# Attention output stored features-first: 1/total spread along TensorE's columns instead of turning tiles in a three-stage float32 kernel

## The chip, the cores and the metric

One NeuronCore of a Trainium2 chip runs the whole program. The metric is the device time of one execution in microseconds, as the median over runs; 1,080.85 us before the change.

## The reference, cut to what matters

Three stages follow each other, all in float32:

```python
# attention: batch 4, heads 8, sequence 576, head size 64
scores = q @ k.T / 8 + bias                      # bias from a small network on positions
attn = exp(scores - max); attn /= attn.sum(-1) + 1e-09
x = (attn @ v) as [2304 tokens, 512 features]    # token = batch*576 + s, feature = head*64 + d
# dense layer, 512 -> 2048 -> 512
h = x @ w_in;  g = h - tanh(h);  x2 = g @ w_out
# routing to one of 8 experts, 512 -> 1024 -> 512
out[token] = gate * (relu(x2 @ w1[e]) @ w2[e])
```

## The kernel before, in words

**Attention.** Two heads at a time form a pair; there are 16 pairs (`PAIRS_A`), and pair `g` belongs to batch `g % 4`. The 576 queries of a pair are five tiles (`QT`): four of 128 and one of 64 (`rows`). The loop over `STEPS` runs one step per pair and tile, written by hand and in software-pipelined order on each engine. In one step TensorE does, in this order: the scores of the next tile (L412, 12 matmuls), the transposes of the probabilities into `pt_a` (L420, four), one slot of the product with v for the pair before (L427, two float32 matmuls of 512 columns, one for each head: the first writes partitions 0 to 63 of the output, the second 64 to 127), the transposes into `pt_b` (four), one `turn_out` (L458), and the transpose of the middle tile of probabilities into `misc`. In the last step of a pair (tile 4) `values_rest` stands between `turn_out` and that last transpose: ten float32 matmuls of 64 columns in the same two-head form.

The product with v leaves the output turned: partitions are the 128 features of the two heads, columns are tokens. VectorE copies it to `o_sb` (`copy_main` L672, `copy_rest` L678). `turn_out` then transposes one tile of `o_sb` into a quarter of the bank `misc`, and `scaled` (L664) multiplies it by 1/total, which `inverse` (L650 to L654) has computed as [token, tile, head], and writes `x_sb`. SyncE stores each pair's `x_sb` in `x_dram` [token, feature] with two DMAs (L368, L369). `misc` has one user at a time: `misc_free` makes TensorE wait for ScalarE's copy of the middle tile, for `copy_rest` and for `scaled`.

**The passage to the dense layer.** After the last step TensorE turns the first chunk of x (`turn_first_x`, L929, 12 transposes into the three free score banks), turns tiles 1 to 4 of pair 14, finishes the product with v for pair 15, does `first_up` (the first two up-projections, L985), turns the five tiles of pair 15, and enters the dense loop.

**Dense layer.** Six chunks of 384 tokens (`CHUNKS`, `CN`), 16 slots each (`FT`, one per 128 of the 2048 hidden features), so 96 slots. In a slot `m` TensorE does up-projection `m + 2` (12 matmuls of 384 columns, L985) and down-projection `m` (9 matmuls of 512 columns, L1042). Every operand is split in a high and a low part; `g` goes ScalarE, VectorE, ScalarE, VectorE before the down-projection may start (L1149 to L1256; `low`, L1230, comes last). At slots 0, 3 and 6 of a chunk (`X_PREP`) `turn_x` transposes one 128-token tile of the next chunk of x (four transposes, L1029); ScalarE and VectorE split it into `xt_hi` and `xt_lo` (L1142, L1235). At slots 1, 3, 5, 7 and 9 of chunk 0 both also split 1 MB of weights (L1178, L1180, `split_w`). x is loaded into `x_nat` by three DMAs per chunk (L891).

**Experts.** Gather, two matmul layers, scatter; not touched, save for the name of a semaphore.

## Time and profile before

| | |
|---|---|
| median of 3 runs | 1080.85 us (1079.69 to 1084.35) |
| profiled execution | 1080.45 us, its span 1078.7 us |
| TensorE matmul busy | 1037.8 us (96%) |
| TensorE weight load busy | 819.0 us (76%) |
| VectorE busy | 680.2 us (63%) |
| ScalarE busy | 626.1 us (58%) |
| GpSimd busy | 91.2 us (8%) |
| mean granted TensorE clock | 0.989 of full speed |

A busy share is a mean over stages with different limits, and matmuls are pipelined, so a busy TensorE is not one at its peak; what a change is worth is read from the distance between the starts of instructions in the stage that it touches. One float32 matmul shows as two records in the trace; a float32 transpose, or a matmul of rounded (fp32r) operands, as one.

### The profile page before, as it was taken

The page shows a single profiled execution, that of the slowest core. Times are in us where ns is not written, and L with a number is a line of the kernel's source. Part 1 is how long each engine was busy: PE and PEld are TensorE (multiplying, and loading weights), DVE is VectorE, ACT ScalarE, POOL GpSimd, SP SyncE. Part 2 cuts the span into 40 slices and gives each one's busy share as a digit, 9 for nine tenths or more (in the row PEclk, how much of TensorE's full clock was granted, in tenths as well). Part 3 has the DMA queues.
Part 4 walks back from the last instruction along what each step waited for, and adds up shares of the span by engine and source line. Part 5 has one row for each costly group of instructions (what it writes and reads, how often), then busy time and mean ns, then how long its engine had stood idle before and what let it go on. Part 6 is the DMA issues. An engine that isn't in the chain of part 4 may idle for free. (4 is left out here: it accounts for less than half of the span.)

```text
span 1078.7 us, 19176 instructions
## 1 busy us (share of the span) xinstructions
PE 1037.8 (96%) x6642; PEld 819.0 (76%) x6642; DVE 680.2 (63%) x1544; ACT 626.1 (58%) x1331; POOL 91.2 (8%) x134
## 2 busy tenths in 40 slices
PE   5879999999999999999999999999999999999995
PEld 2246666666665899999999999999987888888884
DVE  7967777777787796656657657668753452631410
ACT  6977777777787676655556556556631442622321
POOL 0000000000000000000100100001021331331311
PEclk9999999999999999999999999999989999999998
DMA  6772252431503430000000100201115351531110
GB/s 215 263 243 57 56 177 68 165 84 51 167 24 103 166 108 30 1 30 30 31 1 30 31 1 30 79 30 47 48 40 191 127 200 39 198 110 40 36 47 25
DMA packets 69043, 92.14 MB, mean 85 GB/s; under 512 B 25035, under 2 KB 36683, under 8 KB 68939
## 3 DMA queue, kind: packets, MB, share of 16 engines
q1 hardware_dynamic: 63706, 79.32, 22.5%
q0 software_dynamic: 4192, 11.07, 3.1%
q8 instruction: 51, 0.84, 0.3%
q10 hardware_dynamic: 1056, 0.61, 0.2%
q14 instruction: 38, 0.30, 0.1%
HBM read 66.19 MB, written 25.73 MB: 85 GB/s over the span
## 5 line engine op out<-in xcount | busy, mean ns | idle before, releaser
L985 PE MATMUL score<-dl_xt,dl_weights 128*128 128x384 f32 x1152 | 220.6, 339 | 0.0
L985 PEld LDWEIGHTS score<-dl_xt,dl_weights 128*128 128x128 f32 x1152 | 201.9, 188 | 5.0
L563 ACT ACTIVATE at_prob<-at_neg,at_negmax 128x576 f32<-128x576 f32 (+1 forms) x160 | 123.8, 774 | 52.7 <-DVE at_negmax L644 43.6
L1149 ACT ACTIVATE dl_val<-score 128x384 f32<-128x384 f32 x96 | 47.1, 491 | 145.6 <-PE score L985 144.9
L1239 DVE SCALAR_TENSOR_TENSOR dl_sq<-dl_sq,dl_val 128x384 f32<-128x384 f32 x96 | 53.5, 557 | 111.6 <-ACT dl_sq L1151 111.5
L644 DVE CUSTOM_DVE_ANT_0 at_neg<-score,at_bias 128x576 f32<-128x576 f32 (+1 forms) x160 | 113.9, 748 | 5.6 <-PE score L412 5.3
L1764 PE MATMUL o_acc<-dl_weights,ex_ht_hi 128*128 128x512 f32 (+1 forms) x336 | 108.9, 405 | 1.9 <-DVE ex_ht_lo L1855 1.9
L1733 PE MATMUL score<-dl_weights,ex_xt_hi 128*128 128x512 f32 x336 | 107.3, 401 | 1.4 <-DVE ex_xt_lo L1855 1.4
L427 PE MATMUL o_acc<-at_prob_t,at_v_nat 128*64 128x512 f32 (+1 forms) x320 | 85.7, 616 | 1.2 <-DVE at_o_sb L672 1.2
L1448 POOL DMA_INDIRECT slot_dram<-slot_rows,slot_i x18 | 18.1, 1006 | 750.4 <-DVE slot_i L1320 746.0
L420 PEld LDWEIGHTS pt_b<-id_sb,at_prob 128*128 128x128 f32 (+1 forms) x320 | 32.4, 141 | 63.2 <-ACT at_prob L563 47.8
L1764 PEld LDWEIGHTS o_acc<-dl_weights,ex_ht_hi 128*128 128x128 f32 x336 | 62.5, 191 | 16.0 <-issue 2.1
L1733 PEld LDWEIGHTS score<-dl_weights,ex_xt_hi 128*128 128x128 f32 x336 | 62.7, 192 | 14.0 <-DVE ex_xt_lo L1855 1.8
L1855 DVE TENSOR_TENSOR ex_ht_lo<-pt_b,ex_ht_hi 128x512 fp32r<-128x512 f32 x21 | 14.5, 691 | 89.8 <-ACT ex_ht_hi L1804 89.8
L1816 ACT ACTIVATE ex_y_sb<-o_acc,dl_tile_rows 128x512 f32<-128x512 f32 x21 | 14.4, 688 | 97.1 <-PE o_acc L1764 97.1
L1764 PE MATMUL o_acc<-dl_weights,ex_ht_lo 128*128 128x512 f32 (+1 forms) x168 | 66.8, 398 | 0.0
L1733 PE MATMUL score<-dl_weights,ex_xt_lo 128*128 128x512 f32 x168 | 66.4, 395 | 0.0
L412 PE MATMUL score<-at_k_hi,at_q_hi 64*128 64x288 f32 x320 | 58.6, 342 | 4.8 <-DVE at_negmax L644 3.2
L1042 PE MATMUL o_acc<-dl_weights,dl_g_hi 128*128 128x512 f32 x192 | 60.3, 395 | 2.5 <-DVE dl_g_lo L1230 2.5
L1151 ACT ACTIVATE dl_sq<-dl_val,minus_b 128x384 f32<-128x384 f32 x96 | 59.3, 618 | 3.1
L1042 PE MATMUL score<-dl_weights,dl_g_hi 128*128 128x512 f32 x192 | 59.8, 392 | 0.0
L1250 DVE COPY_PREDICATED dl_sq<-dl_over,dl_big 128x384 f32<-128x384 uint32 x96 | 57.7, 601 | 3.3
(214 smaller groups left out, 2123.5 us busy)
## 6 DMA issues: line engine op xcount, KB each, us to landing
dl_raw<-in_moe_w SPq DMA_DIRECT2D x12, 1024.0 KB, 7.0
ex_raw_b<-in_moe_w SPq DMA_DIRECT2D x8, 1024.0 KB, 6.3
at_bias<-bias_dram SPq DMA_DIRECT2D x3, 2304.0 KB, 10.1
bias_dram<-at_prob SPq DMA_DIRECT2D x20, 288.0 KB, 2.1
at_k_all<-in_k SPq DMA_DIRECT2D x16, 288.0 KB, 3.5
at_q_all<-in_q SPq DMA_DIRECT2D x16, 288.0 KB, 4.3
at_v_nat<-in_v SPq DMA_DIRECT2D x16, 288.0 KB, 3.1
bias_dram<-at_rows_sb SPq DMA_DIRECT2D x16, 288.0 KB, 3.7
```

Of the source, the lines that this page charges most:

```text
L412: last = nc.tensor.matmul(score[c][:, half, 0:HALF], a[g % 2][part, cols], b[g % 2][part, keys], start=i == 0, stop=i == 2)
L427: last = nc.tensor.matmul(o[c * D:(c + 1) * D, at:at + queries.stop - queries.start], v_nat[g % NV][keys, j, :], prob_t[g % 2][keys, j, qu ...
L563: nc.scalar.activation(prob[n % 2][0:m, c, :], neg[c][n % 2][0:m, :], ACT.Exp, bias=negmax[c][n % 2][0:m, 0:1], scale=-1.0, accum_out=tota ...
L644: nc.vector.tensor_tensor_reduce(out=neg[c][n % 2][0:m, :].rearrange("p (a c) -> p a c", a=2), in0=score[c][0:m, :, 0:HALF], in1=bias[hp % ...
L985: last = nc.tensor.matmul(h_ps[m % NHB][:, 0:CN], w[f // KT][:, k, fc], x[c % 2][:, k, :], start=k == 0 and n == 0, stop=k == KT - 1 and n ...
L1042: last = nc.tensor.matmul(x2_ps[j][:, :], g[m % 2][:, tok], w[f // KT][:, f % KT, :], start=f == 0 and n == 0, stop=f == FT - 1 and n == 2)
L1149: nc.scalar.activation(val[m % 2][:, :], h, ACT.Square).then_inc(act_step, 1)
L1151: nc.scalar.activation(sq[m % 2][:, :], val[m % 2][:, :], ACT.Square, bias=minus_b[:, 0:1], scale=SQ_A).then_inc(sq_done, 1)
L1239: nc.vector.scalar_tensor_tensor(out=sq[m % 2][:, :], in0=sq[m % 2][:, :], scalar=SQ_C, in1=val[m % 2][:, :], op0=ALU.add, op1=ALU.mult).t ...
L1250: nc.vector.copy_predicated(s[:, :], over[m % 2][:, :].bitcast(mybir.dt.uint32), big[m % 2][:, :]).then_inc(dve_step, 1)
L1733: last = nc.tensor.matmul(h_ps[half][:, :], x[:, k, :], w1_of(r, half, w)[:, k, :], start=k == 0 and n == 0, stop=k == KT - 1 and n == 2)
L1764: last = nc.tensor.matmul(y_ps[:, :], x[:, half * KT + k, :], w2_of(half, w, k), start=half == 0 and k == 0 and n == 0, stop=half == 1 and ...
```

## The change

x is kept with features on rows all the way. `turn_out` becomes `turn_inverse`: in the same place of TensorE's order, two float32 matmuls per tile instead of one transpose. The stationary operand is one column of 1/total read 64 times (step 0), the moving one the identity, so each lays 1/total of one head along the columns of 64 partitions. `scaled` multiplies `o_sb` by it. `x_dram` becomes [feature, token]; the store is one DMA per pair, the load one DMA per chunk, straight into the form the up-projection wants. `turn_first_x` and `turn_x` are gone; ScalarE and VectorE split x from SBUF (`split_x_high`, `split_x_low`). `load_x` of a later chunk waits for `xt_ready` where it waited for `turned`.

```diff
-        x_sb = [buf(f"x_sb{i}", [P, QT, 2 * D]) for i in range(2)]
+        x_sb = [buf(f"x_sb{i}", [P, QT * 2 * D])[:, 0:S] for i in range(2)]
...
-        x4 = x_dram[0:TOK, :].rearrange("(b s) (c e) -> b c s e", b=NB, e=2 * D)
+        x4 = x_dram.rearrange("(c e) (b s) -> b c e s", b=NB, e=2 * D)
...
-                    dst = x4[p % NB, p // NB]
-                    sp.dma_start(dst[0:MAIN, :].rearrange("(t p) d -> p t d", p=P), x_sb[p % 2][:, 0:QT - 1, :]).then_inc(x_out[p % 2], 16)
-                    sp.dma_start(dst[MAIN:S, :], x_sb[p % 2][0:LAST, QT - 1, :]).then_inc(x_out[p % 2], 16)
+                    sp.dma_start(x4[p % NB, p // NB], x_sb[p % 2]).then_inc(x_out[p % 2], 16)
...
-            def turn_out(p, tile, bank, at):
+            def turn_inverse(p, tile, bank, at):
+
                 if tile == 0:
-                    pe.wait_ge(o_read, p + 1)
-                if tile == QT - 1:
-                    pe.wait_ge(rem_read, p + 1)
+                    pe.wait_ge(norm_step, 2 * p + 2)
                 m = rows(tile)
-                nc.tensor.transpose(bank[0:m, at:at + P], o_sb[:, tile * P:tile * P + m], id_sb[:, :]).then_inc(turn_done, 1)
+                for c in range(2):
+                    one = inv[p % 2][0:m, tile, c:c + 1]
+                    many = bass.AP(one.tensor, one.offset, [one.ap[0], [0, D]])
+                    last = nc.tensor.matmul(bank[c * D:(c + 1) * D, at:at + m], many, id_sb[0:m, 0:m], start=True, stop=True)
+                last.then_inc(turn_done, 1)
...
-            dense.turn_first_x(pe)
             misc_free(PAIRS_A, 0)
             for tile in range(1, QT - 1):
-                turn_out(LASTP - 1, tile, misc, tile * P)
+                turn_inverse(LASTP - 1, tile, misc, tile * P)
...
             def scaled(p, tile, tiles, bank, at):
...
-                dve.wait_ge(norm_step, 2 * p + 2)
                 dve.wait_ge(turn_done, QT * p + tile + tiles)
...
+                dve.wait_ge(o_read, p + 1)
+                if tile + tiles == QT:
+                    dve.wait_ge(rem_read, p + 1)
+                nc.vector.tensor_tensor(x_sb[p % 2][:, cols], o_sb[:, cols], bank[:, at:at + m], ALU.mult).then_inc(x_done, tiles)
...
         def load_x(sp, c):
-            for j in range(CH):
-                sp.dma_start(x_nat[:, j, :], x_tiles[c, :, j, :]).then_inc(x_in[j], 16)
+            sp.dma_start(x_t, x_dram[:, c * CN:(c + 1) * CN].rearrange("(k p) t -> p k t", p=P)).then_inc(x_in, 16)
...
         def load_second_x(sp):
-            sp.wait_ge(turned, CH)
+            sp.wait_ge(xt_ready, CH)
             load_x(sp, 1)
...
+        def split_x_high(act, c, j):
             cols = slice(j * P, (j + 1) * P)
+            act.wait_ge(x_in, 16 * (c + 1))
+            if c >= 2:
+                act.wait_ge(h_done, FT * (c - 1))
+            nc.scalar.activation(xt_hi[c % 2][:, :, cols], x_t[:, :, cols], ACT.Copy).then_inc(xt_high, 1)
+
+        def split_x_low(dve, c, j):
+            cols = slice(j * P, (j + 1) * P)
+            dve.wait_ge(xt_high, c * CH + j + 1)
+            nc.vector.tensor_tensor(xt_lo[c % 2][:, :, cols], x_t[:, :, cols], xt_hi[c % 2][:, :, cols].bitcast(F32),
                                     ALU.subtract).then_inc(xt_ready, 1)
...
                 down(m)
-                j = x_prep(m)
-                if j is not None:
-                    if m == 0:
-                        attention.turned(pe)
-                    turn_x(m // FT + 1, j)
                 j = x2_turn(m)
...
-    x_dram = scratch("x_dram", (TOK, DM))
+    x_dram = scratch("x_dram", (DM, TOK))
```

In the order of the built programs, TensorE, one step of the attention loop from the `pt_a` transposes on (output<-operands, size, how many in a row; `at_inv` is 1/total). Before:

```order
L420 MATMUL pt_a<-id_sb,at_prob 128x128 x4
L427 MATMUL o_acc<-at_prob_t,at_v_nat 64x512 x2
L420 MATMUL pt_b<-id_sb,at_prob 128x128 x4
L458 MATMUL misc<-id_sb,at_o_sb 128x128
L420 MATMUL misc<-id_sb,at_prob 128x128
```

and now:

```order
L416 MATMUL pt_a<-id_sb,at_prob 128x128 x4
L423 MATMUL o_acc<-at_prob_t,at_v_nat 64x512 x2
L416 MATMUL pt_b<-id_sb,at_prob 128x128 x4
L456 MATMUL misc<-id_sb,at_inv 64x128 x2
L416 MATMUL misc<-id_sb,at_prob 128x128
```

One transpose among transposes has become two matmuls of 64 partitions, in the same place. TensorE again, from the last step of attention into the dense loop. Before:

```order
L458 MATMUL misc<-id_sb,at_o_sb 128x128
L427 MATMUL misc<-at_prob_t,at_v_nat 64x64 x10
L420 MATMUL misc<-id_sb,at_prob 128x64
L929 MATMUL score<-id_sb,dl_x_nat 128x128 x12
L458 MATMUL misc<-id_sb,at_o_sb 128x128 x3
L458 MATMUL pt_a<-id_sb,at_o_sb 64x128
L427 MATMUL o_acc<-at_prob_t,at_v_nat 64x512 x8
L427 MATMUL pt_b<-at_prob_t,at_v_nat 64x64 x10
L985 MATMUL score<-dl_xt,dl_weights 128x384 x24
L458 MATMUL misc<-id_sb,at_o_sb 128x128 x4
L458 MATMUL pt_a<-id_sb,at_o_sb 64x128
L985 MATMUL score<-dl_xt,dl_weights 128x384 x12
```

and now:

```order
L456 MATMUL misc<-id_sb,at_inv 64x128 x2
L423 MATMUL misc<-at_prob_t,at_v_nat 64x64 x10
L416 MATMUL misc<-id_sb,at_prob 128x64
L456 MATMUL misc<-id_sb,at_inv 64x128 x6
L456 MATMUL pt_a<-id_sb,at_inv 64x64 x2
L423 MATMUL o_acc<-at_prob_t,at_v_nat 64x512 x8
L423 MATMUL pt_b<-at_prob_t,at_v_nat 64x64 x10
L974 MATMUL score<-dl_xt,dl_weights 128x384 x24
L456 MATMUL misc<-id_sb,at_inv 64x128 x8
L456 MATMUL pt_a<-id_sb,at_inv 64x64 x2
L974 MATMUL score<-dl_xt,dl_weights 128x384 x12
```

The 12 transposes of the first chunk, which stood ahead of the first reuse of `misc`, are gone, and the turns of pairs 14 and 15 are twice as many instructions. TensorE, end of slot 0 of the dense loop. Before:

```order
L1042 MATMUL pt_b<-dl_weights,dl_g_hi 128x512 x2
L1042 MATMUL pt_b<-dl_weights,dl_g_lo 128x512
L1042 MATMUL score<-dl_weights,dl_g_hi 128x512 x2
L1042 MATMUL score<-dl_weights,dl_g_lo 128x512
L1029 MATMUL misc<-id_sb,dl_x_nat 128x128 x4
L985 MATMUL score<-dl_xt,dl_weights 128x384 x12
```

and now:

```order
L1020 MATMUL pt_b<-dl_weights,dl_g_hi 128x512 x2
L1020 MATMUL pt_b<-dl_weights,dl_g_lo 128x512
L1020 MATMUL score<-dl_weights,dl_g_hi 128x512 x2
L1020 MATMUL score<-dl_weights,dl_g_lo 128x512
L974 MATMUL score<-dl_xt,dl_weights 128x384 x12
```

The four transposes are gone here and in 14 more slots; nothing stands in their place.

## Rows read from the trace of the kernel before

**Rows 1.** Stretches: engine busy us (instructions), granted clock, DMA share, GB/s

```profile
98.00:344.00 246.00, 244.25 (x2106) 153.19 (x2106) 193.12 (x573) 185.07 (x521) 0.00 (x0) 1.00 0.34 100
360.00:762.00 402.00, 401.50 (x2137) 365.24 (x2138) 275.26 (x553) 249.45 (x497) 14.25 (x15) 1.00 0.12 41
```

**Rows 2.** Timeline, TensorE matmuls, attention: start us, us, engine, line, count

```profile
301.65 0.40 PE L412 MATMUL score<-at_k_hi,at_q_hi 64*128 64x288 f32 x2
...
305.15 0.40 PE L412 MATMUL score<-at_k_hi,at_q_hi 64*128 64x288 f32 x2
...
312.34 0.40 PE L412 MATMUL score<-at_k_hi,at_q_hi 64*128 64x288 f32 x2
...
315.73 0.40 PE L412 MATMUL score<-at_k_hi,at_q_hi 64*128 64x288 f32 x2
...
319.16 0.40 PE L412 MATMUL score<-at_k_hi,at_q_hi 64*128 64x288 f32 x2
```

**Rows 3.** The same timeline, one step from its `pt_a` transposes on

```profile
309.94 0.65 PE L420 MATMUL pt_a<-id_sb,at_prob 128*128 128x128 f32 x4
310.53 1.08 PE L427 MATMUL o_acc<-at_prob_t,at_v_nat 128*64 128x512 f32 x4
311.54 0.66 PE L420 MATMUL pt_b<-id_sb,at_prob 128*128 128x128 f32 x4
312.03 0.27 PE L458 MATMUL misc<-id_sb,at_o_sb 128*128 128x128 f32 x1
312.14 0.27 PE L420 MATMUL misc<-id_sb,at_prob 128*128 128x128 f32 x1
```

**Rows 4.** The same, a narrow window at 310.5 us: the first two of those four L427

```profile
310.53 0.65 PE L427 MATMUL o_acc<-at_prob_t,at_v_nat 128*64 128x512 f32 x2
```

**Rows 5.** The same timeline, last step of a pair

```profile
307.75 0.33 PE L458 MATMUL misc<-id_sb,at_o_sb 128*128 128x128 f32 x1
308.01 0.95 PE L427 MATMUL misc<-at_prob_t,at_v_nat 128*64 128x64 f32 x20
308.88 0.27 PE L420 MATMUL misc<-id_sb,at_prob 64*128 64x64 f32 x1
```

**Rows 6.** Timeline, TensorE, attention into the dense layer

```profile
344.44 1.53 PE L929 MATMUL score<-id_sb,dl_x_nat 128*128 128x128 f32 x12
345.80 0.49 PE L458 MATMUL misc<-id_sb,at_o_sb 128*128 128x128 f32 x3
...
346.33 3.80 PE L427 MATMUL o_acc<-at_prob_t,at_v_nat 128*64 128x512 f32 x16
...
355.21 0.60 PE L458 MATMUL misc<-id_sb,at_o_sb 128*128 128x128 f32 x4
...
360.50 0.70 PE L1042 MATMUL o_acc<-dl_weights,dl_g_hi 128*128 128x512 f32 x2 [2.47 <-DVE dl_g_lo L1230]
```

**Rows 7.** Timeline, VectorE, the same stretch

```profile
345.01 0.21 DVE L678 COPY at_o_sb<-misc 128x64 f32<-128x64 f32 x1
...
355.95 0.69 DVE L664 TENSOR_TENSOR at_x_sb<-misc,at_inv 128x512 f32<-128x512 f32 x1 [3.77 <-PE pt_a L458]
```

**Rows 8.** Timeline, TensorE, first slots of the dense layer

```profile
362.62 0.60 PE L1029 MATMUL misc<-id_sb,dl_x_nat 128*128 128x128 f32 x4
...
367.25 2.27 PE L985 MATMUL score<-dl_xt,dl_weights 128*128 128x384 f32 x12
369.35 0.62 PE L1042 MATMUL o_acc<-dl_weights,dl_g_hi 128*128 128x512 f32 x2
...
371.43 2.27 PE L985 MATMUL score<-dl_xt,dl_weights 128*128 128x384 f32 x12
```

**Rows 9.** Timeline, VectorE, the low part for the down-projection at 369.35

```profile
368.58 0.55 DVE L1230 TENSOR_TENSOR dl_g_lo<-dl_val,dl_g_hi 128x384 fp32r<-128x384 f32 x1
```

**Rows 10.** Timeline, SyncE: the issues of the second load of x

```profile
349.75 1.71 SPq L891 DMA_DIRECT2D dl_x_nat<-x_dram  x3
```

**Rows 11.** Timeline, ScalarE: the first split of the second chunk of x

```profile
365.08 0.59 ACT L1142 ACTIVATE dl_xt<-misc 128x512 fp32r<-128x512 f32 x1
```

More of the change, by code:

```diff
@@ L119 @@
     x2_copied: object
-    turned: object
+    xt_ready: object
     scattered: object
@@ L502, in tensor @@
                 if turn_of(g, t):
-                    turn_out(*turn_of(g, t), misc, TURN_AT)
+                    turn_inverse(*turn_of(g, t), misc, TURN_AT)
                 if t == QT - 1 and real(g - 1):
@@ L520, in tensor @@
             for tile in range(QT - 1):
-                turn_out(LASTP, tile, misc, tile * P)
-            turn_out(LASTP, QT - 1, pt_a, 0)
+                turn_inverse(LASTP, tile, misc, tile * P)
+            turn_inverse(LASTP, QT - 1, pt_a, 0)
         def scalar(act, dense):
@@ L608, in scalar @@
             for j in range(CH):
[L609 removed]
+                dense.split_x_high(act, 0, j)
             dense.split_second_high(act)
@@ L732, in vector @@
             for j in range(CH):
-                dense.split_first_x_low(dve, j)
+                dense.split_x_low(dve, 0, j)
             dense.split_second_low(dve)
@@ L828, in dense_and_routing @@
         route = mem.pt_a
-        first_turn = [h.rearrange("p (k t) -> p k t", t=P) for h in halves[0:CH]]
+        x_t = x_nat[:, :, :].rearrange("p j n -> p (j n)").rearrange("p (k t) -> p k t", t=CN)
         raw_in = [sem(f"raw_in{i}") for i in range(2)]
@@ L836, in dense_and_routing @@
         slots_cleared = sem("slots_cleared")
-        x_in = [sem(f"x_in{j}") for j in range(CH)]
-        turned, xt_high, xt_ready = sem("turned"), sem("xt_high"), sem("xt_ready")
+        x_in, xt_high, xt_ready = sem("x_in"), sem("xt_high"), sem("xt_ready")
         const_set, ones_set = sem("const_set"), sem("ones_set")
@@ L923, in set_constants @@
             nc.vector.memset(seen[:, :], 0.0).then_inc(seen_set, 1)
-        def turn_first_x(pe):
-            for j in range(CH):
-                pe.wait_ge(x_in[j], 16)
-                for k in range(KT):
-                    last = nc.tensor.transpose(first_turn[j][:, k, :], x_nat[:, j, k * P:(k + 1) * P], id_sb[:, :])
-                last.then_inc(turned, 1)
-        def split_first_x_high(act, j):
-            act.wait_ge(turned, j + 1)
-            nc.scalar.activation(xt_hi[0][:, :, j * P:(j + 1) * P], first_turn[j][:, :, :], ACT.Copy).then_inc(xt_high, 1)
-        def split_first_x_low(dve, j):
-            dve.wait_ge(xt_high, j + 1)
-            cols = slice(j * P, (j + 1) * P)
-            nc.vector.tensor_tensor(xt_lo[0][:, :, cols], first_turn[j][:, :, :], xt_hi[0][:, :, cols].bitcast(F32),
+        def split_x_high(act, c, j):
+            cols = slice(j * P, (j + 1) * P)
+            act.wait_ge(x_in, 16 * (c + 1))
[6 more added lines that the diff above has]
+            nc.vector.tensor_tensor(xt_lo[c % 2][:, :, cols], x_t[:, :, cols], xt_hi[c % 2][:, :, cols].bitcast(F32),
                                     ALU.subtract).then_inc(xt_ready, 1)
@@ L1020, in tensor @@
         def tensor(pe, experts):
-            def turn_x(c, j):
-                n = c * CH + j
-                pe.wait_ge(x_in[j], 16 * (c + 1))
-                if n:
-                    pe.wait_ge(xt_ready, n)
-                if j == 0 and c >= 3:
-                    pe.wait_ge(x2_copied, CH * (c - 2))
-                for k in range(KT):
-                    last = nc.tensor.transpose(turn[:, k, :], x_nat[:, j, k * P:(k + 1) * P], id_sb[:, :])
-                last.then_inc(turned, 1)
             def down(m):
@@ L1077, in tensor @@
                 down(m)
-                j = x_prep(m)
-                if j is not None:
-                    if m == 0:
-                        attention.turned(pe)
-                    turn_x(m // FT + 1, j)
                 j = x2_turn(m)
                 if j is not None:
+                    if m // FT == 1 and j == 0:
+                        attention.turned(pe)
                     if j == 0:
-                        if m // FT < LATE:
-                            pe.wait_ge(xt_ready, CH * (m // FT + 2))
                         pe.wait_ge(x2_read[0], m // FT)
@@ L1139, in scalar @@
         def scalar(act, experts):
-            def split_x(c, j):
-                act.wait_ge(turned, c * CH + j + 1)
-                nc.scalar.activation(xt_hi[c % 2][:, :, j * P:(j + 1) * P], turn[:, :, :], ACT.Copy).then_inc(xt_high, 1)
             def polynomial(m):
@@ L1647, in first_gather @@
             pool.wait_ge(dense.scattered, 16 * CH * FULL_CHUNKS)
-            pool.wait_ge(dense.turned, NTT)
+            pool.wait_ge(dense.xt_ready, NTT)
             nc.gpsimd.dma_start(early_slots, slot_dram.rearrange("(p n) c -> p n c", p=P)).then_inc(early_slots_in, 16)
```

51 lines of the change are left out of this document (19 added, 32 removed).

## The prediction

> **What bounds the kernel now.** I read the busy time by stretches first [rows 1]. In attention TensorE has a matmul under way in 244.25 of 246 us, VectorE is busy for 193 and ScalarE for 185. In the dense layer it is 401.5 of 402, against 275 and 249. So in both stages that the change touches TensorE sets the pace, its clock is granted in full, and DMA has room (share 0.34 and 0.12). Then the timeline of TensorE in attention. Steps of equal content start 3.50, 3.39 and 3.43 us apart (301.65 to 305.15, 312.34 to 315.73, 315.73 to 319.16), and a pair of five steps takes 17.51 [rows 2]. Inside a step nothing stands still: what an instruction costs is the distance to the next start [rows 3]. The step of 3.50 and the one of 3.43 hold 0.15 us more than the shortest; I read that as short waits, which added work on TensorE can fill. The stretch between attention and the dense layer is different: there TensorE waits 2.47 us for the first activation [rows 6].
>
> So the change is a trade on one engine: it takes transposes away from the dense layer and makes the turns in attention dearer.
>
> **What it removes.** In the dense layer 15 groups of four transposes go. A slot with such a group lasts 362.62 to 367.25 = 4.63 us, one without 367.25 to 371.43 = 4.18 [rows 8]. The group costs 0.45, and 15 of them 6.75 us. Of this not all comes through: in chunk 0 VectorE is loaded with the weight splits, and the low part for the down-projection at 369.35 is done at 368.58 + 0.55 = 369.13, only 0.22 earlier [rows 8, 9]. TensorE gains 0.45 before that slot, so 0.23 is lost there, and something like it may happen again behind the splits at slots 3 to 9. The whole gain of chunk 0 is 1.35, so 0.23 to 1.35 is lost; I take 0.65. **Dense layer: -6.1 us** (-5.4 to -6.5).
>
> The 12 transposes of the first chunk take 345.80 - 344.44 = 1.36 us [rows 6]. That is inside the passage and is summed there.
>
> **What it makes dearer.** A turn in attention now costs the distance 312.03 to 312.14, 0.11 us [rows 3]. In its place come two float32 matmuls, four records. The trace has none of this size, so I build the price from two neighbours of the same form (two heads, 64 output partitions each): the values matmuls of 512 columns and the rest of 64 columns.
>
> - The four records of 512 columns take 310.53 to 311.54 = 1.01 us to the next start [rows 3]. The first two of them end 0.43 us before the last two (1.08 - 0.65) [rows 3, 4]: two records, one on each half of the output, stream side by side, 512 columns in 0.43, which is 0.84 ns per column. Shortened to 128 columns, each half loses 384 columns or 0.32 us: 1.01 - 0.645 = 0.365 us. To 64 columns: 0.26.
> - Entering such a group from transposes costs extra: the last of the four `pt_a` transposes starts at 309.94 + 0.65 - 0.27 = 310.32, the next matmul 0.21 later, where a transpose follows after 0.11 [rows 3]. So 0.10 more.
> - From both sides: the least is pure streaming, 2 x 0.107 = 0.215 for 128 columns, with no cost of entering or leaving. The most, if the two heads did not stream side by side, is 4 x 0.107 plus the 0.15 that the 512-column group spends beyond its streaming (1.01 - 0.86), 0.58. The row nearest in form is the 512-column group, so I take 0.365 with the 0.10.
>
> Per pair, then. Steps 0 to 2, tiles 1 to 3: 0.365 + 0.10 - 0.11 = 0.36 each, 1.07. Step 3, the 64-token tile: 0.26 + 0.10 - 0.11 = 0.25. Step 4, where tile 0 is followed by the rest: now the turn costs 308.01 - 307.75 = 0.26, the entering included [rows 5]; a string of 64-column groups takes 0.87 / 5 = 0.175 each, which is 0.07 over its streaming, so a 128-column group in a string is 0.285, with the 0.10 0.385: +0.12. Together 1.44 per pair, less the 0.15 of waits that it can fill, **1.29 per pair**. Fourteen pairs are turned wholly inside the steps: **+18.1 us** (least 0.43 per pair, 6.0; with nothing filled 1.44, 20.2).
>
> By the Trainium skill ("TensorE: Matmul & The Clock Gate", The mechanism, and LDWEIGHTS) a weight load hides under running matmuls only if it is in other rows of the array, and takes a time in proportion to its columns, some 53 ns for 64. Both heads use all rows here, so by that rule (an estimate) the four loads would lie open, 0.43 us for the group and 0.06 more per tile. The trace disagrees: 20 loads and 20 matmuls of 64 columns fit in 0.87 us, 44 ns for both together [rows 5].
>
> **The passage.** Before, the 12 transposes hid a wait: the next turns need `misc`, which VectorE frees with `copy_rest`, ending at 345.01 + 0.21 = 345.22 [rows 7]; TensorE came at 345.80 [rows 6]. Without them it stands from 344.5 on until about 345.4 (0.12 later from step 4 included), so of 1.36 only 0.4 is won. Three turns in a string at 0.285 and the small one at 0.18 are 1.03, and the values matmuls start at 346.45, against 346.33 [rows 6]. They are of the same form, so nothing is paid for the change of form. Everything is 0.12 late up to the turns of pair 15, which began at 355.21 [rows 6]. Four groups of 0.285 instead of four transposes end 0.8 later, and VectorE's `scaled`, at 355.95 before [rows 7], would start at about 356.85. On it hangs the chain to the first down-projection at 360.50, where TensorE was waiting anyway [rows 6]. **Passage: +0.9 us** (0.5 to 1.5), pair 14's last turns and pair 15's included.
>
> **What costs nothing.** `scaled` multiplies the same number of elements on VectorE, from SBUF and a bank instead of a bank and SBUF; the 64-token tile becomes 64 columns instead of 128. ScalarE and VectorE split x from SBUF instead of from a bank. If either were dearer by a tenth, it is covered by their idle quarter and more [rows 1], save in chunk 0 where the loss above stands. VectorE's `copy_main` and `copy_rest` now wait for VectorE's own `scaled`, which precedes them in its order. DMA: the store is one issue of 2,304-byte rows where there were two issues with 512-byte rows, the load one issue where there were three. SyncE is no bound. The second load must wait for the split of the first chunk. It is issued at 349.75 now [rows 10], and the split that it feeds comes at 365.08 [rows 11]: 15 us of cover. If that were gone, ScalarE would stand in front of the activation of slot 2, and TensorE with it.
>
> **Sum.** 1080.45 + 18.1 + 0.9 - 6.1 = 1093.35 for the profiled execution. The median of the runs shown is 0.4 above that execution's time, so I predict **1093.7 us**, 1.2% slower. About 0.5% (5.4 us) is what a measurement of this kernel can tell from no change.
>
> **Rivals.**
> - *The turns cost only their streaming* (not slower). Four records of 128 columns slip between the transposes at 0.215, with no price for entering and leaving. Then 0.105 x 4 = 0.43 per pair, 6.0 for fourteen; the passage about +0.3; dense in full, -6.75: 1080.4, no change. For it: in a string of 64-column groups nearly nothing is spent beyond streaming [rows 5]. Against it: the 0.21 and the 1.01 of [rows 3]. It decides below 0.76 us per pair, where the sum comes under 5.4. Chance 0.14; a gain over 0.5% needs an addition below zero per pair, and I give 0.03 for what I have not seen, a stall in attention that goes with the changed waits.
> - *The two heads do not stream side by side*, say because a column read 64 times loads otherwise than the real weights of the rows. Tile 0.58: three times 0.57, for the 64-token tile 4 x 0.054 + 0.15 + 0.10 - 0.11 = 0.36, step 4 about 0.40: 2.5 per pair, 35; passage +2.5; 1080.85 + 37.5 - 6.1 = 1112. For it: no row shows such an operand. Against: the form is that of the values matmuls. Chance 0.07.
> - *The weight loads lie open.* If all loads of 64 columns show, at about the 44 ns that a load and a matmul have now [rows 5] and beside the 0.107 of streaming, a group is 0.39 to 0.43, 1.5 to 1.7 per pair and nothing filled: +21 to +24, passage +1.3: 1097 to 1100. This is also where the rule above leads. Chance 0.11.
> - *ScalarE waits for x* at slot 1 of the dense layer, or a chunk's load comes late each time: 1 to 3 us on top. Chance 0.03.
>
> **How the numbers follow.** The case of the sum has 0.62; its own bounds (1.15 to 1.44 per pair, passage and dense by theirs) give 1091 to 1097. Both slower rivals and the late load add 0.21. The no-change case has 0.14 and a gain 0.03. The range 1083 to 1101 holds the case of the sum and of the open loads, and a weak form of the first rival; outside lie most of the no-change case and the 1112, together a little under 0.2. Faster by over 0.5%: 0.03. Within 0.5%: 0.14. Slower: 0.83.
>
> **What would show it.** Steps 0 to 2 should last about 3.75 us where the shortest lasted 3.39, with the middle transpose starting some 0.37 after the first matmul of `turn_inverse`, and a pair 18.8 instead of 17.51. TensorE should stay busy throughout attention, with VectorE and ScalarE idling more. The dense slots should all last 4.18, with a wait of a few tenths before a down-projection in chunk 0. Before the turns of pair 14 TensorE should stand for about 0.9 us. The experts should last as before. I am wrong if a pair takes less than 18.3 or more than 19.2, if the dense loop is not shorter by 5 us, or if ScalarE waits for `x_nat`.

## The result, and the profile after

| | before | changed | ratio |
|---|---|---|---|
| at the prediction | 1081.71 us (1079.69 to 1084.35, 4 runs) | 1093.1 us (1091.89 to 1094.93, 4 runs) | 1.0105, 95% interval 1.0077 to 1.0133 |
| once more, later | 1081.11 us (29 runs) | 1093.19 us (6 runs) | 1.0113, 95% interval 1.0094 to 1.0131 |
| profiled execution | 1080.45 us, span 1078.7 | 1094.93 us, span 1093.2 | |

The change makes the kernel 1.1% slower, 11.4 to 12.1 us. The prediction was 1093.7 us.

Stretches of the changed kernel, in the columns of [rows 1] (us; busy time of PE, PEld, DVE, ACT, POOL; granted clock, DMA share, GB/s), for attention and for the dense layer:

```profile
98.00:362.00 264.00, 263.67 (x2318) 160.09 (x2316) 192.53 (x573) 192.54 (x521) 0.00 (x0) 1.00 0.30 94
380.00:776.00 396.00, 396.00 (x2077) 359.95 (x2076) 274.38 (x552) 248.22 (x494) 14.09 (x15) 1.00 0.13 41
```

TensorE is busy almost without a gap in both, as before. In attention VectorE is busy for 73% of the stretch instead of 79%, ScalarE for 73% instead of 75%. The timeline of TensorE, one whole step with the neighbours that answer to [rows 3] and [rows 5] (start, us, engine, line, count):

```profile
304.56 0.46 PE L416 MATMUL pt_b<-id_sb,at_prob 64*128 64x64 f32 x4
304.94 0.44 PE L456 MATMUL misc<-id_sb,at_inv 128*64 128x128 f32 x4
305.21 0.90 PE L423 MATMUL misc<-at_prob_t,at_v_nat 128*64 128x64 f32 x20
...
306.05 0.45 PE L408 MATMUL score<-at_k_hi,at_q_hi 64*128 64x288 f32 x2
...
307.67 1.08 PE L423 MATMUL o_acc<-at_prob_t,at_v_nat 128*64 128x512 f32 x4
308.68 0.65 PE L416 MATMUL pt_b<-id_sb,at_prob 128*128 128x128 f32 x4
309.26 0.44 PE L456 MATMUL misc<-id_sb,at_inv 128*64 128x128 f32 x4
309.63 0.33 PE L416 MATMUL misc<-id_sb,at_prob 128*128 128x128 f32 x1
309.89 0.40 PE L408 MATMUL score<-at_k_hi,at_q_hi 64*128 64x288 f32 x2
```

Three distances are longer than in [rows 3]: from the `pt_b` transposes to the turn 0.58 instead of 0.49, the turn itself 0.37 (309.26 to 309.63) instead of 0.11, from the middle transpose to the next scores 0.26 (309.63 to 309.89) instead of 0.20. In the last step of a pair (the first lines) the turn takes 0.27, against 0.26 before. This step lasts 306.05 to 309.89 = 3.84. All five, start of scores to start of scores:

| us per step | 0 | 1 | 2 | 3 | 4 | pair |
|---|---|---|---|---|---|---|
| before | 3.45 | 3.39 | 3.43 | 3.50 | 3.74 | 17.51 |
| changed | 3.85 | 3.79 | 3.80 | 3.68 | 3.73 | 18.85 |
| difference | 0.40 | 0.40 | 0.37 | 0.18 | -0.01 | 1.34 |

The passage and the first slots of the dense layer, on TensorE, where [rows 6] and [rows 8] stood:

```profile
363.44 0.87 PE L456 MATMUL misc<-id_sb,at_inv 128*64 128x128 f32 x12 [0.97 <-DVE at_o_sb L675]
364.25 0.33 PE L456 MATMUL pt_a<-id_sb,at_inv 64*64 64x64 f32 x4
364.51 3.80 PE L423 MATMUL o_acc<-at_prob_t,at_v_nat 128*64 128x512 f32 x16
...
373.49 1.09 PE L456 MATMUL misc<-id_sb,at_inv 128*64 128x128 f32 x16
374.51 0.33 PE L456 MATMUL pt_a<-id_sb,at_inv 64*64 64x64 f32 x4
374.77 2.37 PE L974 MATMUL score<-dl_xt,dl_weights 128*128 128x384 f32 x12
379.29 0.80 PE L1020 MATMUL o_acc<-dl_weights,dl_g_hi 128*128 128x512 f32 x2 [2.15 <-DVE dl_g_lo L1199]
379.89 0.63 PE L1020 MATMUL o_acc<-dl_weights,dl_g_lo 128*128 128x512 f32 x1
...
382.88 2.41 PE L974 MATMUL score<-dl_xt,dl_weights 128*128 128x384 f32 x12
```

Before the turns of pair 14 TensorE now stands for 0.97 us. At the first down-projection the records last longer than in [rows 6], 0.63 where 0.39 stood: the granted clock is below full there. The rows of this stretch, first of the kernel before, then of the changed one:

```profile
360.00:381.50 21.50, 21.00 (x109) 19.02 (x110) 19.91 (x32) 17.73 (x32) 0.00 (x0) 1.00 0.49 159
```

```profile
379.00:400.50 21.50, 21.21 (x98) 18.85 (x99) 19.05 (x31) 17.12 (x31) 0.00 (x0) 0.92 0.52 158
```

The two profiled spans, cut at the same instructions, differ by 14.5 us:

| stretch | before | changed | difference |
|---|---|---|---|
| start to the first scores | 98.78 | 98.73 | -0.05 |
| 68 steps of attention | 238.45 | 256.50 | +18.05 |
| last scores to the first down-projection | 23.27 | 24.06 | +0.79 |
| to the end of the last down-projection | 430.99 | 426.10 | -4.89 |
| experts | 287.21 | 287.81 | +0.60 |

### The profile page after: what moved, and what is told of

Read it like the earlier page. It is cut to its first block and busy times, and to the rows that moved or that the text cites. A ratio compares the mean times of both kernels' runs of the same rounds, so it can differ in the third digit from the quotient of the medians.

```text
span 1093.2 us, 19491 instructions
## 1 busy us (share of the span) xinstructions
PE 1052.0 (96%) x6810; PEld 820.9 (75%) x6810; DVE 679.7 (62%) x1544; ACT 633.3 (58%) x1331; POOL 91.7 (8%) x134
## 5 line engine op out<-in xcount | busy, mean ns | idle before, releaser
L1819 DVE TENSOR_TENSOR ex_ht_lo<-pt_b,ex_ht_hi 128x512 fp32r<-128x512 f32 x21 | 14.5, 691 | 89.8 <-ACT ex_ht_hi L1768 89.8
```

## The experiments

All edits are made to the changed kernel; the kernel before stood beside each group of runs at 1081.0 to 1081.1 us. The expectations name runs by their labels, which stand in brackets here.

**1. One wide transpose per tile** (e1_wide_transpose). VectorE writes 1/total 64 times (640 elements where it wrote 10), and a tile is turned by one float32 transpose.

```diff
-                for c in range(2):
-                    one = inv[p % 2][0:m, tile, c:c + 1]
-                    many = bass.AP(one.tensor, one.offset, [one.ap[0], [0, D]])
-                    last = nc.tensor.matmul(bank[c * D:(c + 1) * D, at:at + m], many, id_sb[0:m, 0:m], start=True, stop=True)
-                last.then_inc(turn_done, 1)
+                many = inv[p % 2][0:m, tile, :, :].rearrange("p c d -> p (c d)")
+                nc.tensor.transpose(bank[:, at:at + m], many, id_sb[0:m, 0:m]).then_inc(turn_done, 1)
```

> 1/total is written 64 times by the reciprocal on VectorE (640 elements per partition instead of 10), and each tile is one float32 transpose of that 128-column tile, one record, where the changed kernel has two matmuls, four records. Theory (TensorE pays for the four records, for entering and for leaving a group of float32 matmuls): the transpose costs 0.11 us as the turn before did, a pair falls from 18.84 back to about 17.5, VectorE hides its added 0.6 us per pair; 1093.1 - 14 x 1.33 - 0.7 in the passage = 1073.8, range 1072 to 1077, so faster than the kernel before by the dense layer's transposes. Rival (a pair is longer for another reason than these records, for example because scaled now reads o_sb from SBUF and a bank, or through the changed waits): a pair stays above 18, the kernel above 1081.

Measured: 1173.88 us, 1.086 (1.0845 to 1.0875), where 1073.8 was expected. The reciprocal was priced wrongly, at 0.6 us more per pair. VectorE's groups and TensorE's waits in attention (group: busy us, mean ns; wait: us in total, times, longest):

```profile
L650 DVE RECIPROCAL at_inv<-at_guarded 128x640 f32<-128x640 f32 x10 | 41.5, 4153 | 0.3
```

```profile
PE misc L454 <- DVE at_x_sb L662: 27.4, 10, 2.7
PE score L408 <- DVE at_negmax L639: 7.0, 10, 0.8
```

It takes 4.15 us where it took 0.217 for 10 elements, so 3.9 more per pair, and TensorE waits 3.4 us for VectorE in each pair. That is only part of the loss, since a pair takes 23.90 instead of 17.51, 6.4 more. The rest goes with the clock: from 100 to 340 us the granted clock is 0.86, where the kernel before has 1.00 in attention. The 0.14 that is missing, of 23.9 us, makes 3.3 us (an estimate). In the pair that waits until 285.70 us the clock is 0.50 from 286 to 292 us, the lower of its two levels (1.2 instead of 2.4 GHz), and back at 1.00 from 294 on. The steps outside that stall are clean, 3.45 and 3.39, the turn again 0.11: 299.92 to 300.03.

**2. One wide matmul per tile** (e2_one_wide). The same wide 1/total, but a matmul of 128 stationary columns (two records) in place of the transpose. The diff is against run 1.

```diff
-                nc.tensor.transpose(bank[:, at:at + m], many, id_sb[0:m, 0:m]).then_inc(turn_done, 1)
+                nc.tensor.matmul(bank[:, at:at + m], many, id_sb[0:m, 0:m], start=True, stop=True).then_inc(turn_done, 1)
```

> The same wide 1/total, but each tile is one float32 matmul of 128 stationary columns: two records that use the whole width, instead of four that use a half each. Theory (the two heads stream side by side, so the four records take the time of two): no change, the group stays 0.35 to 0.37 to the next start, total 1091 to 1095. Rival (the halves take turns, and four records cost four): the group falls to about 0.22, three tiles save 0.15 each and a pair 0.55, total about 1085.

Measured: 1170.8 us, 1.0839 (1.0822 to 1.0856), with the same reciprocal and a granted clock of 0.90 in attention, so the time decides nothing. An undisturbed step:

```profile
301.14 0.66 PE L416 MATMUL pt_b<-id_sb,at_prob 128*128 128x128 f32 x4
301.63 0.39 PE L454 MATMUL misc<-id_sb,at_inv 128*128 128x128 f32 x2
301.85 0.27 PE L416 MATMUL misc<-id_sb,at_prob 128*128 128x128 f32 x1
```

The prediction put the 0.10 of entering down to the change from transposes to matmuls. Here a matmul follows transposes at 0.49, as a transpose did, and gives way after 0.22. It pays neither for entering nor for leaving. The theory of this run, 0.35 to 0.37 for the group, fell. The rival's 0.22 came, though not for its reason, since run 3 shows the halves side by side.

So what the changed kernel's turn pays goes with two matmuls of half the width, one on each half of the output partitions. The width alone does not explain it. In step 3 the kernel before turns its 64-token tile with a transpose of 128 rows that fills only 64 output partitions (128*64), also among full-width transposes:

```profile
304.23 0.66 PE L420 MATMUL pt_b<-id_sb,at_prob 128*128 128x128 f32 x4
304.72 0.27 PE L458 MATMUL misc<-id_sb,at_o_sb 128*64 128x128 f32 x1
304.83 0.27 PE L420 MATMUL misc<-id_sb,at_prob 128*128 128x128 f32 x1
305.15 0.40 PE L412 MATMUL score<-at_k_hi,at_q_hi 64*128 64x288 f32 x2
```

It enters at 0.49 and gives way after 0.11, like a full one, and so do all 13 of its kind between 100 and 335 us. Whether the price belongs to half-width matmuls, as against transposes, or to the use of both halves, no run separates.

**3. The two matmuls of a turn issued twice** (e3_twice).

```diff
-                for c in range(2):
+                for c in (0, 1, 0, 1):
```

> The two matmuls of every tile are issued twice in a row. Theory (most of the price is entering and leaving; within a string a group of 128 columns costs 0.27 to 0.285 and one of 64 columns 0.17): 4 x 0.28 + 0.17 = 1.3 us more per pair, 14 pairs 18, passage 2: total 1110 to 1114. Pure streaming (0.215 and 0.107) gives 13.6 and 1.5: 1108. Rival (the whole 0.52 of a group, from the last transpose before to the first score after, belongs to the group itself): 4 x 0.47, 26 and more: above 1119.

Measured: 1109.28 us, 1.0273 (1.0257 to 1.0288).

```profile
323.14 0.66 PE L456 MATMUL misc<-id_sb,at_inv 128*64 128x128 f32 x8
323.73 0.33 PE L416 MATMUL misc<-id_sb,at_prob 128*128 128x128 f32 x1
```

Eight records take 0.59, so the second four cost 0.22. That is the pure streaming of the prediction's lower bound (0.215): weight loads included, the two halves run side by side and nothing is added. So the turn's 0.37 is 0.22 of streaming and 0.15 that is paid once per group. By the Trainium skill ("TensorE: Matmul & The Clock Gate", The mechanism) loads overlap a running matmul only where the row groups differ. Here they are the same, and the four loads show nowhere. The same section also lets a load into the background weight buffer run ahead, which would fit; no run here tells.

**4. The turn behind the values matmuls** (e4_after_values), ahead of the `pt_b` transposes, in steps 0 to 3: one change of form less, since the values matmuls also come in two halves of 64 partitions.

```diff
                     values_main(g - 1, t + 1)
+                if t < QT - 1:
+                    misc_free(g, t)
+                    if turn_of(g, t):
+                        turn_inverse(*turn_of(g, t), misc, TURN_AT)
...
                 last.then_inc(ptb_done, 1)
-                misc_free(g, t)
-                if turn_of(g, t):
-                    turn_inverse(*turn_of(g, t), misc, TURN_AT)
+                if t == QT - 1:
+                    misc_free(g, t)
+                    if turn_of(g, t):
+                        turn_inverse(*turn_of(g, t), misc, TURN_AT)
```

> In steps 0 to 3 the two matmuls stand right behind the values matmuls, ahead of the pt_b transposes, so that the form of the work changes no further time. Theory (entering 0.09, leaving 0.06 and the unhidden end of the group are paid only between matmuls and transposes): tiles 1 to 3 cost about 0.27 instead of 0.52, the small one 0.17 instead of 0.41, 0.9 to 1.0 us less per pair: total 1079 to 1082. Rival (the earlier place waits for misc, which ScalarE and VectorE have not freed yet, or the price does not depend on the neighbours): 1088 or more, in the first case with waits on scaled in front of the group.

Measured: 1080.27 us over 10 runs, 0.9993 (0.9982 to 1.0003).

```profile
303.54 1.08 PE L423 MATMUL o_acc<-at_prob_t,at_v_nat 128*64 128x512 f32 x4
304.45 0.39 PE L456 MATMUL misc<-id_sb,at_inv 128*64 128x128 f32 x4
304.77 0.66 PE L416 MATMUL pt_b<-id_sb,at_prob 128*128 128x128 f32 x4
```

Values and turn together take 303.54 to 304.77 = 1.23, where the values alone took 1.01 [rows 3]: the turn costs its 0.22. A pair takes 17.80 (3.55, 3.51, 3.54, 3.50, 3.70), 1.05 less than in the changed kernel. Moving one call takes back the whole loss. It does not make the kernel faster: a pair is still 0.29 longer than before, and its 68 steps take 4.8 us more, as much as the dense layer gains in its profiled execution (426.10 against 430.99).

**5 and 6. Real columns without the long reciprocal** (e5_widen_pool, e6_widen_dve). 1/total stays narrow; a copy widens it, on GpSimd once per pair (5) or on VectorE one tile per step (6); a tile is one transpose.

```diff
+                many = wide[p % 2][0:m, tile, :, :].rearrange("p c d -> p (c d)")
+                nc.tensor.transpose(bank[:, at:at + m], many, id_sb[0:m, 0:m]).then_inc(turn_done, 1)
...
+                nc.gpsimd.tensor_copy(wide[p % 2][:, :, :, :].rearrange("p t c d -> p (t c) d"), many).then_inc(widened, 1)
```

> The reciprocal stays at 10 elements; GpSimd, idle in attention, copies 1/total of a pair 64 times (640 elements per partition) and each tile is one transpose of that tile. Theory: the steps return to 3.39 to 3.50 and a pair to 17.5, as the undisturbed steps of the run with the wide reciprocal (3.39 and 3.45) already show; 1093.1 - 14 x 1.33 - 0.7 = 1073.8, range 1072 to 1077. Rival: VectorE slows down beside GpSimd, or the copy comes too late for tile 0: a pair of 18 or more, above 1080, with longer VectorE instructions or a wait on GpSimd in front of the turn.

> The same, but VectorE widens one tile per step by a copy of 128 elements, behind scaled. Theory: 0.2 to 0.28 us more on VectorE per step fit in its idle time, 17.5 to 17.7 per pair, 1073 to 1078. Rival: VectorE's chain to the scores of the next tile is the next bound (the 0.15 us per pair of waits in the kernel before), a pair takes 18 or more and the kernel over 1081, with TensorE waiting for the negated scores.

Measured: 5 1081.02 us, 0.9998 (0.9984 to 1.0011); 6 1079.22 us, 0.9983 (0.9971 to 0.9995); 10 runs each. Both missed their ranges, 1072 to 1077 and 1073 to 1078. A copy of the same 640 elements takes 0.72 us on GpSimd, which has nothing else to do there:

```profile
L744 POOL COPY at_wide<-at_inv 128x640 f32<-128x640 f32 x14 | 10.0, 716 | 236.8 <-DVE at_inv L652 236.8
```

Steps 0 to 2 of run 5 are those of the kernel before (3.45, 3.39, 3.43), but step 3 takes 3.63. It turns the 64-token tile:

```profile
307.06 0.66 PE L419 MATMUL pt_b<-id_sb,at_prob 128*128 128x128 f32 x4
307.64 0.27 PE L457 MATMUL misc<-id_sb,at_wide 64*128 64x64 f32 x1
307.84 0.33 PE L419 MATMUL misc<-id_sb,at_prob 128*128 128x128 f32 x1
308.10 0.40 PE L411 MATMUL score<-at_k_hi,at_q_hi 64*128 64x288 f32 x2
```

A single transpose of 64 rows among transposes of 128 has the same marks as the turn of the changed kernel, 0.58 before it and 0.26 behind the next, and itself takes 0.20 instead of 0.11. So a change in the number of rows costs like the changed kernel's change of form.

Step 3 is not all that run 5 lacks. Its profiled execution has the whole gain of the dense layer (424.86 us against 430.99), but its 68 steps take 240.99 against 238.45, and behind the dense layer it is 4.0 longer (291.17 against 287.21), in code that the edit does not touch; the last heading comes back to that. In run 6 a pair takes 17.80, where 17.5 to 17.7 was expected. Step 2 takes 3.56 instead of 3.43: VectorE's extra copies reach TensorE.

**7. The dense layer's transposes put back as dummies** (e7_dense_turns; four transposes of the identity at each of the 15 places).

```diff
                 down(m)
+                if x_prep(m) is not None:
...
+                    for k in range(KT):
+                        nc.tensor.transpose(turn[:, k, :], id_sb[:, :], id_sb[:, :])
```

> The changed kernel with four transposes (of the identity, read by nobody) back at each of the 15 places in the dense loop. Theory: each group costs 0.45 us on TensorE, 6.75 less what VectorE's splits in chunk 0 had swallowed (0.3 to 0.65): 1099.0 to 1100.0. Rival (most of the gain of the dense layer came from elsewhere, for example from splits that no longer wait for TensorE): 1093 to 1096.

Measured: 1099.74 us, 1.0167 (1.0145 to 1.0189), 6.6 us over the changed kernel. From the first down-projection to the end of the last 431.13 us pass, against 430.99 in the kernel before. The dense layer's gain is those transposes and nothing else. This execution has the full clock there.

**8. Twelve dummy transposes before the turns of pair 14** (e8_first_turns), to fill the 0.97 us of waiting.

```diff
+            for j in range(3):
+                for k in range(4):
+                    nc.tensor.transpose(score[j // 2][:, j % 2, k * P:(k + 1) * P], id_sb[:, :], id_sb[:, :])
             misc_free(PAIRS_A, 0)
```

> The changed kernel with 12 transposes of the identity, read by nobody, back between the last step of attention and the turns of pair 14. Theory: TensorE stood about 1 us there waiting for VectorE's copy, so 1.36 us of transposes cost only 0.3 to 0.5: 1093.5, not to be told from 1093.1 by the time; in the timeline the turns of pair 14 begin 0.3 to 0.5 later after the last middle transpose than the 1.24 of the changed kernel, and no wait stands before them. Rival: the wait comes on top, 1.4 us more from the last middle transpose to the first down-projection.

```profile
361.19 1.53 PE L510 MATMUL score<-id_sb 128*128 128x128 f32 x12
362.64 0.88 PE L456 MATMUL misc<-id_sb,at_inv 128*64 128x128 f32 x12
```

The wait is gone and 1.45 us of transposes stand in it; from the last scores to the first down-projection it is 24.47 us instead of 24.06. So of the 12 transposes' 1.45 only 0.41 was ever to be won. The median, 1096.47 us (1.0133, 1.0111 to 1.0156), is 3.3 over the changed kernel's. In the profiled execution of this run the stretch behind the dense layer, which the edit does not touch, takes 290.28 us against 287.81, 2.5 more. That stretch comes back under the last heading.

**9. The 64-row transpose made a 128-row one** in 5 (run 9a, e10_full_rows) and in 6 (run 9b, e12_full_rows_dve); the surplus columns are not read. The edit doubles the rows of this transpose and the columns that it streams together.

```diff
-                many = wide[p % 2][0:m, tile, :, :].rearrange("p c d -> p (c d)")
-                nc.tensor.transpose(bank[:, at:at + m], many, id_sb[0:m, 0:m]).then_inc(turn_done, 1)
+                many = wide[p % 2][:, tile, :, :].rearrange("p c d -> p (c d)")
+                nc.tensor.transpose(bank[:, at:at + P], many, id_sb[:, :]).then_inc(turn_done, 1)
```

> Of e5_widen_pool, only the turn of the 64-token tile is changed: it is a transpose with all 128 rows (128 columns of output, of which 64 are used) and not one with 64 rows. Theory (what costs at the edges of a turn is a change of the size of tile that TensorE works in, rows as well as columns): the step that holds it goes from 3.63 to 3.50 us, the distance from its middle transpose to the next scores from 0.26 to 0.20, a pair from 17.67 to 17.5, fourteen pairs give 1.8 us, about 1079.2 us. Rival (the 64-row transpose is as cheap as any, the 3.63 comes from a wait of VectorE or the like): the step stays at 3.6 or gets longer by the 0.05 of 64 more rows, 1081 to 1082 us.

> The same edit on e6_widen_dve. Theory of the tile size: a pair from 17.80 to 17.65, about 1077.3 us from 1079.2. Rival: unchanged, 1079 to 1080 us. The two versions also tell which engine does the widening more cheaply: in e6 one step of a pair (3.56) was dearer than in e5 (3.43), yet its median was 1.8 us lower; if the difference between the two medians is again there, it is outside the attention steps.

Measured: 9a 1079.05 us, 0.998 (0.9967 to 0.9993); 9b 1079.04 us, 0.9983 (0.997 to 0.9996); 12 runs each. Run 9a:

```profile
304.98 0.66 PE L419 MATMUL pt_b<-id_sb,at_prob 128*128 128x128 f32 x4
305.47 0.27 PE L456 MATMUL misc<-id_sb,at_wide 128*128 128x128 f32 x1
305.58 0.27 PE L419 MATMUL misc<-id_sb,at_prob 128*128 128x128 f32 x1
305.89 0.40 PE L411 MATMUL score<-at_k_hi,at_q_hi 64*128 64x288 f32 x2
```

The expectations of 9a came true in the steps and in the time. A transpose of twice the rows is the cheaper one: the entering is 0.49 again, the turn 0.11, step 3 3.50 and the pair 17.51. One detail missed: the scores follow after 0.31, not 0.20. The kernel before has the same distance in its step 3, 0.32 (304.83 to 305.15 above). It is a wait, which the dearer turn of 5 had filled. In 9b the entering and the turn are 0.49 and 0.11 as well, but the pair stays at 17.8, and the time did not fall to the 1077.3 expected. Its rival, unchanged, came true: in steps 2 and 3 the scores come late (0.38 and 0.45 behind the middle transpose), because TensorE waits for VectorE, which has the extra copies.

```profile
308.16 0.40 PE L410 MATMUL score<-at_k_hi,at_q_hi 64*128 64x288 f32 x2 [0.17 <-DVE at_negmax L639]
```

**10. Real columns as stationary operand** (e9_real_columns): 64 columns of a matrix of ones instead of one column read 64 times.

```diff
-                    one = inv[p % 2][0:m, tile, c:c + 1]
-                    many = bass.AP(one.tensor, one.offset, [one.ap[0], [0, D]])
-                    last = nc.tensor.matmul(bank[c * D:(c + 1) * D, at:at + m], many, id_sb[0:m, 0:m], start=True, stop=True)
+                    last = nc.tensor.matmul(bank[c * D:(c + 1) * D, at:at + m], mem.ones[0:m, c * D:(c + 1) * D], id_sb[0:m, 0:m],
+                                            start=True, stop=True)
```

> Leaves 1/total out: the stationary operand of the turns is 64 real columns of a constant matrix of ones in place of one column of 1/total read 64 times (step 0), all else as in the changed kernel. Theory (such an operand loads like any other): a turn of 128 columns still 0.37 us start to start, a pair 18.8, the median within 1.5 us of the changed kernel's 1093. Rival (the column read 64 times is part of the price, as the prediction's second rival had it): the group falls to 0.3 or less, a pair to 18.5 or less, the median to 1088 or less.

Measured: 1079.98 us, 0.999 (0.9979 to 1.0001), over 12 runs. The median alone would say that the rival won. The trace says otherwise:

```profile
308.86 0.44 PE L454 MATMUL misc<-id_sb,ones 128*64 128x128 f32 x4
309.23 0.33 PE L416 MATMUL misc<-id_sb,at_prob 128*128 128x128 f32 x1
```

The turn is 0.37, and the steps are 3.85, 3.79, 3.80, 3.68, 3.74, those of the changed kernel. Most of the 13 us went from the experts. With 1/total left out x has other values, tokens go to other experts, and one tile of tokens fewer is computed. The experts' output copies on ScalarE, first of this run, then of the changed kernel:

```profile
L1779 ACT ACTIVATE ex_y_sb<-o_acc,dl_tile_rows 128x512 f32<-128x512 f32 x20 | 13.8, 688 | 94.7 <-PE o_acc L1727 94.7
```

```profile
L1780 ACT ACTIVATE ex_y_sb<-o_acc,dl_tile_rows 128x512 f32<-128x512 f32 x21 | 14.4, 688 | 98.8 <-PE o_acc L1728 98.8
```

Tiles start 12.4 us apart. The stretch behind the dense layer is 273.02 us here and 287.81 in the changed kernel, 14.8 less: one tile, and 2.4 in the last tile, where TensorE stands for 1.51 us instead of 2.66 and the clock stays full until its matmuls are done. The operand read 64 times costs nothing extra.

**11. The changed kernel once more** (e11_after_again), as a control.

> The changed kernel once more, as a control on the same chip as the three above. 1093 us within 1.5; its profile should show the dense layer's TensorE clock at 1.00 where the first profile had 0.96 over the first slots (409.0 us there from the first down-projection on would then be 404.6), if that dip belonged to the one execution. e8 was 3.4 us over the changed kernel where its passage was 0.4 longer: if this control comes out at 1096, that difference is between chips and not in e8's edit; if at 1093, e8's 3 us lie in its edit.

Measured: 1093.19 us, 1.0113 (1.0094 to 1.0131), span 1091.5. The half of the expectation on the clock fell. The granted clock behind the first down-projection is 0.92 again, and the dense layer takes 426.05 us:

```profile
377.60:399.10 21.50, 21.17 (x98) 18.89 (x99) 19.07 (x31) 17.16 (x31) 0.00 (x0) 0.92 0.50 157
```

So it is in both profiled executions of the changed kernel, though not in run 10, whose dense layer is the same. The other half of the expectation said that a control at 1093 puts the 3 us of run 8 into that run's edit. The control came out at 1093.19. The trace gives the edit only 0.4 of them, in the passage; 2.7 more than in this control lie behind the dense layer, and the cause of these stays open.

## Why the prediction was right, point by point

- **What bounds.** TensorE in both stages, as read from [rows 1]; it has almost no gap in the changed kernel either (263.67 of 264 us).
- **Streaming side by side.** 0.84 ns per column and record pair, taken from [rows 3, 4], gave 0.365 for the turn; measured 0.37. Run 3 separates it into 0.22 and 0.15.
- **Entering, 0.10.** Measured 0.09. Its cause was named wrongly: a change from transposes to matmuls alone costs nothing (run 2), nor does half the width alone (the 128*64 transpose above). It comes with the pair of half-width matmuls, and nothing narrower is shown.
- **Leaving.** The sum had nothing for it. The next scores start 0.06 later (0.26 instead of 0.20) in steps 0 to 3.
- **Step 4, +0.12.** Measured -0.01. The sum paid the 0.10 of entering here too and took 0.285 for the group. The turn takes 0.27 and is entered at 0.38 (304.56 to 304.94), where the kernel before needs 0.39: the `pt_b` transposes of this step have 64 rows, so a change of size stood in front of the turn before as well, and behind it now stands work of its own form. Two errors largely cancel, and that is luck: four times 0.06 too little, 0.13 too much in step 4.
- **Waits to be filled, 0.15 per pair.** Steps 2 and 3 grew by 0.03 and 0.12 less than their turns. Per pair 1.29 was predicted and 1.34 measured.
- **Passage, +0.9.** Measured +0.49, from the `pt_a` transposes of the last step (at 340.61 and at 358.91) to the first down-projection. What was missed is a wait for `at_o_sb` before pair 15's first values matmul, 0.63 us before and 0.33 now, which the later turn fills by 0.3. The wait before the turns of pair 14 was put at 0.9 and is 0.97; that only 0.4 of the 12 transposes is won, run 8 shows.
- **Dense layer, -6.1.** In run 10, which has the changed kernel's dense layer at full clock, it is 424.89 us against 430.99: -6.10. The loss in chunk 0 is there as well: slots 0 to 2 take 4.26, 4.45 and 4.26 instead of 4.18, slot 8 4.28, together 0.53, where 0.65 was taken. The changed kernel itself gains only 4.89: slot 0 runs at the lower clock and takes 5.83. This term of 1.2 us was in no step of the prediction. One of its own signs of being wrong came up by it: the dense loop was to be shorter by 5 us, and it is by 4.89, or 4.94 in the control.
- **Sum.** Predicted 18.1 + 0.9 - 6.1 = 12.9 over the kernel before. The profiled executions differ by 14.5: the 1.2 of the clock and 0.6 in the experts are what the sum did not have. The medians differ by 11.4 and 12.1, less than the profiled ones, since of the changed kernel's first four runs the profiled one was the longest and the kernel before's lay 1.26 below its median. That the forecast lies within 0.6 us of the median is therefore partly luck; the profiled execution was 1.6 above the sum.
- **Rivals.** The turn at its streaming price is real, but only behind the values matmuls (run 4). The two heads not side by side, and the loads lying open, are excluded by run 3, the operand by run 10. x did not come late: it is issued at 367.37 and ScalarE splits it at 383.86 without a wait.

## What to carry to other kernels

Look at the form of the work next to an instruction on TensorE, its rows and the halves of the output that it writes, and not only at the instruction. Here a float32 group of two matmuls of 64 output partitions each takes 0.22 us beside work of its own width and 0.52 (entering 0.09, the group 0.37, leaving 0.06) between full-width work, and a 128-row transpose of which half is thrown away is cheaper than a 64-row one. Place such a group next to others of its form before looking for a better instruction. Where data decide how much work follows, an experiment that changes the data must be read by stage, not by its total.

## What the runs showed of the hardware that I had not expected

- **The reciprocal.** VectorE takes 4.153 us for 640 elements per partition and 0.217 for 10, 6.25 ns for each further one; GpSimd copies 640 in 0.72 us. The Trainium skill names a reason in "VectorE: DVE Perf Modes" (First, the fixed hardware budget): the divide iterates, with a repeat count of 8. It gives no time, so the trace can agree only in kind: a further element costs 6.25 ns, in GpSimd's copy some 1.1.
- **The clock behind a wait.** TensorE waits 2.0 to 2.5 us for the first activation in every profiled execution. Behind the wait the granted clock is below full in some and not in others. Over 21.5 us it is 1.00 in the kernel before (wait 2.47) and in run 9b (2.46), 1.00 in runs 10 and 7 (2.14), and 0.92 in the changed kernel, its control and run 4 (2.14 to 2.15). It is 0.93 in run 8 (2.15) and in run 9a, where the first records take as long as this, after the same wait as before:

```profile
360.96 1.19 PE L1028 MATMUL o_acc<-dl_weights,dl_g_hi 128*128 128x512 f32 x2 [2.47 <-DVE dl_g_lo L1207]
```

  It costs 1.2 us of the dense layer (426.10 against 424.89 in run 10), 1.1 in run 9a against 9b. The length of the wait does not decide it; what does is open.
- **The last tile of the experts.** Before its down-projection TensorE stands for 1.91 us in the kernel before, 2.66 in the changed one and 5.00 in run 9a. There the clock is 0.66 in the five microseconds that follow:

```profile
1060.09 0.98 PE L1736 MATMUL o_acc<-dl_weights,ex_ht_hi 128*128 x2 [5.00 <-issue]
```

```profile
1060.00:1065.00 5.00, 4.91 (x14) 3.89 (x15) 0.00 (x0) 0.00 (x0) 0.30 (x2) 0.66 0.01 3
```

  No edit touches this code. Behind the dense layer run 9a is 3.7 us longer than the kernel before (290.91 against 287.21), and the standstill is 3.1 of them. In that profiled execution it takes back most of what the best version gains, 5.1 us in the dense layer with attention nearly as fast as before (68 steps in 239.03 us). The medians show 2.1 us (0.2%), less than a measurement of this kernel can tell from no change, though the interval lies below 1. The same standstill is 5.22 us in run 5 and 5.43 in run 1, and behind the dense layer these two take 291.2 and 291.1 us. Run 8 has two, of 2.52 and 1.70 us. In the profiled execution of run 5 it makes up 3.3 of the 4.0 us that the stretch is longer. Run 6, whose attention is slower but whose median is 1.8 lower, has 2.53 us of it and 286.94 for the stretch. Whether it is there in the other executions of a kernel is not shown, and its cause, put down to issue by the profile, was not tried.
